# mLSTM attention and two dense layers on one core: how the first three tiles get their maxima, scores, states and weights

## The chip, the core and the metric

The kernel runs on one core of a Trainium2 chip (trn2). The metric is the device time of one execution in microseconds (us), of which three runs are shown. Below, PE is TensorE (PEld its weight loads), DVE is VectorE, ACT is ScalarE, POOL is GpSimd and SP is SyncE, which only issues transfers. "SPq" marks SP's queue.

## The reference

```python
B, H, S, D = 4, 8, 768, 40          # q, k, v, o_gate: (B, H, S, D); i_gate, f_gate: (B, H, S)
for t in range(S):
    m_new = np.maximum(f_gate[:, :, t] + m, i_gate[:, :, t])
    f_stab, i_stab = np.exp(f_gate[:, :, t] + m - m_new), np.exp(i_gate[:, :, t] - m_new)
    m = m_new
    C = f_stab * C + i_stab * (v_t outer k_t);   n = f_stab * n + i_stab * k_t
    y[:, :, t] = sigmoid(o_t) * (C @ q_t) / np.maximum(np.abs(n . q_t), 1.0)
x = y as (B*S, H*D) = (3072, 320)
x = np.maximum(x @ moe_w_in, 0.0) ** 2 @ moe_w_out            # w_in (320, 2048), w_out (2048, 320)
h = x @ moe2_w_in
out = np.where(h > 0.0, h, np.exp(np.minimum(h, 0.0)) - 1.0) @ moe2_w_out
```

All in float32.

## The kernel before

**Tiles.** The sequence is cut into 6 chunks of 128 steps; chunk c of batch b is tile g = 4c + b, 24 tiles of 128 tokens with 8 heads each. The recurrence is computed chunkwise. For each head there is a row m of running maxima (a scan over the gates on DVE). A tile needs its 8 rows of m on all 128 partitions, 1024 columns, in `wts[g % 3]`. ACT turns them into weights with one Exp of 128x128 for each head (`exponents`), POOL zeroes what lies above the diagonal (`mask`), PE forms the scores k·q (`scores`), DVE multiplies weights by scores (`weigh`), PE multiplies by v (`within`), DVE divides by the denominator and applies the output gate (`finish`), PE transposes the tile (`x1_transposed`), and ACT and DVE split it into a high and a low float32r part (`x_hi`, `x_lo`). The state at a chunk's end is the sum of k times `wv` (v weighted by the last column of the weights, `make_wv` on POOL, `state_added` on PE). Chunk 0 (tiles 0 to 3) has no state coming in; its sum is just copied (`first_state` on ACT). From tile 4 on there are also q and k splits and the state's share.

**Dense layers.** Three tiles (384 tokens) form a block, 8 blocks, two layers: 256 steps, t = 16·block + j, j a slice of 128 of the 2048 hidden columns. A step is `first_product(t)` (8 matmuls of 384 columns), the activation (ACT relu and square to `ghi`, POOL the full square `hact`, DVE the rest `glo`), and three steps later `second_product` (9 matmuls of 320 columns). PE's order is written out by hand, so is every other engine's; each engine runs its list in order and waits at semaphores.

**Prologue and block 0.** Tiles 0 to 2 must be done before step 0, since block 0 is made of them. The tiles of the next block are worked on between the steps of a block: tile g begins at step `start_of(g)` (tiles 3, 4, 5 and 6 at steps 0, 5, 10 and 15), with its matmuls at fixed offsets (scores at 0, state at 2, `within` at 3, transpose at 5).

**Weights.** Slice n of the first layer comes by SP as 128x704 words (352 KB) into a ring of four places. ACT makes the high part (`split_hi`, `split_out_hi`), DVE the low part of w_in (`split_lo`, two instructions) and POOL the low part of w_out (`split_out_lo`). Slices 0 to 3 are split in the prologue, slice t + 4 in step t. SP issues the load of slice n only when slice n - 4 is split, and that load stands in SP's list among the loads of q and k, v and the state, each with waits of its own.

**Maxima of the first tiles.** `spread_m` makes the rows of tiles 0 to 2 on PE: the maxima (32 rows) are multiplied with an identity column or with ones into PSUM, in the banks `acc` and `att`. Tiles from 3 on get them by a transfer: the maxima are written to DRAM (`m_rows`) and read back with the rows repeated on all partitions (`load_m`).

## Time and profile before

| | us |
|---|---|
| median of 3 runs | 877.79 (877.78 to 878.11) |
| the profiled execution | 878.74 |
| its span, first to last instruction | 877.0 |
| PE busy | 858.6 (98%) |
| DVE, ACT, POOL busy | 514.6, 436.7, 379.0 |

The span and the profiled time are 1.74 us apart. The stages are: the prologue up to step 0 at 50.73 us, block 0 up to 125.10 us, block 1 up to 183.37 us, and the other fourteen blocks. A row of the profile's views gives start and duration, engine, line of the kernel, operation, what it writes and reads, and at the end in brackets how long its engine had been idle and what released it.

### The profile page before, as it was taken

The page shows a single profiled execution, that of the slowest core. Times are in us where ns is not written, and L with a number is a line of the kernel's source. Part 1 is how long each engine was busy: PE and PEld are TensorE (multiplying, and loading weights), DVE is VectorE, ACT ScalarE, POOL GpSimd, SP SyncE. Part 2 cuts the span into 40 slices and gives each one's busy share as a digit, 9 for nine tenths or more (in the row PEclk, how much of TensorE's full clock was granted, in tenths as well). Part 3 has the DMA queues.
Part 4 walks back from the last instruction along what each step waited for, and adds up shares of the span by engine and source line. Part 5 has one row for each costly group of instructions (what it writes and reads, how often), then busy time and mean ns, then how long its engine had stood idle before and what let it go on. Part 6 is the DMA issues. An engine that isn't in the chain of part 4 may idle for free.

```text
span 877.0 us, 15290 instructions
## 1 busy us (share of the span) xinstructions
PE 858.6 (98%) x5633; PEld 838.5 (96%) x5633; DVE 514.6 (59%) x879; ACT 436.7 (50%) x955; POOL 379.0 (43%) x409
## 2 busy tenths in 40 slices
PE   9996899999999999999999999999999999999998
PEld 7876899999999999999999999999999999999998
DVE  4478888777678587775763764444444444444443
ACT  2274566465565565655734654434444443434343
POOL 2155564454444444543532754333334343433333
PEclk9997999999999999999999999999999999999999
DMA  6265443335354333453402410000000000000000
GB/s 166 82 213 178 133 104 100 99 104 135 90 162 108 101 99 100 108 135 102 130 4 96 117 50 1 16 10 13 11 2 23 1 23 1 24 1 23 1 24 24
DMA packets 21487, 63.86 MB, mean 73 GB/s; under 512 B 3012, under 2 KB 8996, under 8 KB 18852
## 3 DMA queue, kind: packets, MB, share of 16 engines
q1 hardware_dynamic: 21412, 62.88, 25.7%
q8 instruction: 45, 0.74, 0.4%
q14 instruction: 30, 0.25, 0.1%
HBM read 55.61 MB, written 4.03 MB: 68 GB/s over the span
## 4 chain that ended last, share of the span: by engine, by line
PE 91%; DVE 5%; DMA 1%; issue 1%; ACT 1%; POOL 1%; SPq 0%; DVEq 0%; ACTq 0%; POOLq 0%
PE hps L932 39%; PE acc L946 37%; PE att L849 4%; PE att L798 2%; PE att L841 2%; PE att L832 1%; PE att L854 1%; DMA x<-in_w_all 1%; PE acc L819 1%; DVE win L652 1%; PE hps L877 1%; PE att L855 1%; DVE win L651 1%; PE hps L798 0%; PE acc L807 0%
## 5 line engine op out<-in xcount | busy, mean ns | idle before, releaser
L932 PE MATMUL hps<-xth,win 128*128 128x384 f32 x1280 | 351.5, 340 | 2.2 <-DVE xtl L644 1.2
L946 PE MATMUL acc<-wout,ghi 128*128 128x320 f32 x1536 | 348.5, 313 | 0.0
L932 PE MATMUL hps<-xtl,win 128*128 128x384 f32 x768 | 260.2, 339 | 0.0
L946 PEld LDWEIGHTS acc<-wout,ghi 128*128 128x128 f32 x1536 | 259.0, 189 | 0.3 <-POOL glo L377 0.3
L946 PE MATMUL acc<-wout,glo 128*128 128x320 f32 x768 | 238.2, 310 | 0.0
L932 PEld LDWEIGHTS hps<-xth,win 128*128 128x128 f32 x1280 | 230.4, 189 | 3.0 <-DVE xtl L644 1.6
L377 POOL TENSOR_TENSOR glo<-hact,ghi 128x384 fp32r<-128x384 f32 x128 | 130.0, 1016 | 218.6 <-ACT ghi L544 218.6
L370 POOL TENSOR_TENSOR hact<-hact 128x384 f32<-128x384 f32 x128 | 109.5, 855 | 182.1 <-ACT hact L499 180.1
L748 DVE TENSOR_TENSOR glo<-hact,ghi 128x384 fp32r<-128x384 f32 x128 | 81.3, 635 | 116.1 <-POOL hact L370 115.8
L499 ACT ACTIVATE hact<-hps 128x384 f32<-128x384 f32 x128 | 62.7, 490 | 169.9 <-PE hps L932 169.9
L932 PEld LDWEIGHTS hps<-xtl,win 128*128 128x128 f32 x768 | 145.2, 189 | 0.0
L946 PEld LDWEIGHTS acc<-wout,glo 128*128 128x128 f32 x768 | 144.7, 188 | 0.0
L539 ACT ACTIVATE hact<-hact 128x384 f32<-128x384 f32 x128 | 67.3, 526 | 132.1 <-DVE hact L767 132.1
L767 DVE TENSOR_SCALAR hact<-hps 128x384 f32<-128x384 f32 x128 | 71.2, 556 | 104.0 <-PE hps L932 104.0
L770 DVE SCALAR_TENSOR_TENSOR hact<-hact,hps 128x384 f32<-128x384 f32 x128 | 70.9, 554 | 76.7 <-ACT hact L539 76.7
L544 ACT ACTIVATE ghi<-hact 128x384 fp32r<-128x384 f32 x128 | 67.2, 525 | 74.4 <-DVE hact L770 74.4
L502 ACT ACTIVATE ghi<-hact 128x384 fp32r<-128x384 f32 x128 | 67.1, 525 | 4.0
L301 POOL TENSOR_TENSOR q<-raw,q 40x512 fp32r<-40x512 f32 x40 | 57.4, 1453 | 11.2 <-ACT q L394 11.2
L418 ACT ACTIVATE wts<-wts,a_col 128x128 f32<-128x128 f32 x168 | 53.1, 388 | 0.0
L574 DVE RECIPROCAL gate<-gate 128x320 f32<-128x320 f32 x24 | 51.7, 2153 | 0.8
L849 PEld LDWEIGHTS att<-kvo,wts 128*128 128x128 f32 x352 | 43.9, 198 | 1.5 <-issue 1.5
L849 PE MATMUL att<-kvo,wts 128*128 128x41 f32 x352 | 43.0, 284 | 0.0
(151 smaller groups left out, 736.3 us busy)
## 6 DMA issues: line engine op xcount, KB each, us to landing
raw<-in_qk SPq DMA_DIRECT2D x20, 960.0 KB, 7.1
kvo<-in_kvo SPq DMA_DIRECT2D x23, 484.0 KB, 7.8
wts<-m_rows SPq DMA_DIRECT2D x21, 512.0 KB, 4.8
x<-in_w_all SPq DMA_DIRECT2D x16, 352.0 KB, 6.4
wts<-in_w_all SPq DMA_DIRECT2D x12, 352.0 KB, 3.0
out_x<-hsum SPq DMA_DIRECT2D x16, 160.0 KB, 1.9
state_rows<-state SPq DMA_DIRECT2D x40, 52.5 KB
kvo<-in_w_all SPq DMA_DIRECT2D x4, 352.0 KB, 4.4
```

Source lines behind the costliest of these rows:

```text
L370: nc.gpsimd.tensor_tensor(gfull[t % 2], relu[t % 2], relu[t % 2], ALU.mult).then_inc(s["g_ready"], 1)
L377: nc.gpsimd.tensor_tensor(glo[t % GR][:], gfull[t % 2], f32(ghi[t % GR][:]), ALU.subtract)\
L499: nc.scalar.activation(relu[t % 2], hps[t % 2][:, 0:NT], ACT.Relu).then_inc(s["relu_ready"], 1)
L502: nc.scalar.activation(ghi[t % GR][:], relu[t % 2], ACT.Square).then_inc(s["ghi_ready"], 1)
L539: nc.scalar.activation(relu[t % 2], relu[t % 2], ACT.Exp).then_inc(s["e_ready"], 1)
L544: nc.scalar.activation(ghi[t % GR][:], gfull[t % 2], ACT.Copy).then_inc(s["ghi_ready"], 1)
L748: nc.vector.tensor_tensor(glo[t % GR][:], gfull[t % 2], f32(ghi[t % GR][:]), ALU.subtract)\
L767: nc.vector.tensor_scalar(relu[t % 2], hps[t % 2][:, 0:NT], 0.0, None, ALU.min).then_inc(s["hneg_ready"], 1)
L770: nc.vector.scalar_tensor_tensor(out=gfull[t % 2], in0=relu[t % 2], scalar=-1.0, in1=hps[t % 2][:, 0:NT], op0=ALU.add, op1=ALU.max).then_i ...
L849: last = nc.tensor.matmul(bank[:, h * E:(h + 1) * E], wts[g % 3][:, h, :], v_of(g)[:, h, :], start=True, stop=True)
L932: last = nc.tensor.matmul(hps[t % 2][:, 0:NT], win[:, j, w, :], x[:, kk, :], start=(i == 0), stop=(i == len(parts) - 1))
L946: last = nc.tensor.matmul(acc[u][:, 0:DM], g[t % GR][:, cols], wout[:, j, w, :], start=(j == 0 and i == 0), stop=(j == NF - 1 and i == 2))
```

## The change

- Tiles 0 to 2 get their maxima by the transfer through DRAM too. `spread_m` and the `pick_m` of POOL are gone. ACT's `exponents` read them in place from `wts`.
- PE's prologue is in another order: the scores of tiles 0, 1 and 2 stand ahead of all `within`. Tile 2's scores go to `acc[0]`, `acc[1]`. The chunk-boundary maxima and the transposes of the inner part go to the free bank `acc[2]` instead of `hps[0]` and `att`. Of the 13 warming matmuls 8 are left, all at the start (before: 9, 1 and 3).
- `state_added(2)` moves from the prologue to step 1, `state_added(3)` to step 3; the last columns of the weights are kept by POOL (`keep_last`) and not by DVE, in one buffer for each tile.
- Tile 3 starts at step 1, tile 4 at 6, tile 5 at 11; tile 6 stays at 15.
- The ring has six places (`RING = 6`); slices 0 to 5 are split ahead of step 0 (`EARLY = 6`), their low part of w_in on POOL; in step t slice t + 6 is split. Slices 12 to 15 are loaded from ACT's queue in steps 2 to 5. SP issues slices 0 to 11 ahead of its step list. k, v and o of tiles 2 and 3 get buffers of their own.
- The output gate's 1 + e is made by ACT (Copy with bias) and not by DVE. `finish` stands one step earlier, behind `glo`.

```diff
-RING = 4
+RING = 6
+EARLY = 6
+POOL_LO = 6
+FROM_ACT = 12
+BEHIND = 2
+FIRST_STATES = {1: 2, 3: 3}
 def start_of(g):
-    return NF * (g // T - 1) + 5 * (g % T) - (g >= 2 * T)
+    if g < 2 * T:
+        return (1, 6, 11)[g - T]
+    return NF * (g // T - 1) + 5 * (g % T) - 1
...
+        def load_w(eng, n):
+            slot, loaded, _ = raw_w(n)
+            if n == RING - 3:
+                wait(eng, "s_ps", 4)
+            before = n - RING if n < NF else n - SPARE if n >= NF + SPARE else -1
+            if before >= 0:
+                win_lo_done(eng, before)
+                wait(eng, "wout_lo", before + 1)
+            eng.dma_start(slot, w_all[n // NF, n % NF]).then_inc(loaded, 16)
...
             for t in range((BLOCKS - 1) * NF):
-                if t + RING < NF:
-                    load_w(t + RING)
...
-            mask(0)
-            make_wv(0)
...
+            for g in range(T):
+                mask(g)
+                keep_last(g)
+                if g == 0:
+                    make_wv(0)
+            for n in range(EARLY):
+                if n == 4:
+                    make_wv(1)
+                    mask(T)
+                    keep_last(T)
+                if n < POOL_LO:
+                    split_lo(n)
+                split_out_lo(n)
             make_wv(2)
...
+            exponents(2, 1)
+            out_gate(1)
+            out_gate(2)
+            for n in range(2):
+                split_hi(n)
+                split_out_hi(n)
+            x_hi(0, 0, 0, A0)
+            for n in range(2, 4):
+                split_hi(n)
+                split_out_hi(n)
+            x_hi(1, 0, 1, A0)
+            first_state(0)
+            exponents(3, 0)
+            x_hi(2, 0, 2, A0)
+            exponents(3, 1)
+            first_state(1)
+            for n in range(4, EARLY):
+                split_hi(n)
+                split_out_hi(n)
+            out_gate(3)
...
-                        if t + RING < NF:
-                            split_hi(t + RING)
-                            split_out_hi(t + RING)
+                        if t + EARLY < NF:
+                            split_hi(t + EARLY)
+                            split_out_hi(t + EARLY)
+                        if FROM_ACT <= t + RING + EARLY - BEHIND < NF:
+                            load_w(act, t + RING + EARLY - BEHIND)
...
-                        g = tile_at(t, 4)
-                        if g is not None:
-                            finish(g)
...
+                        if t + EARLY < NF:
+                            split_lo(t + EARLY)
+                        g = tile_at(t, 3)
+                        if g is not None:
+                            finish(g)
```

PE's list from the first transpose to tile 2's scores (`ident` identity matrix, `raw` and one part of `x` hold q and k). Before:

```order
L883 MATMUL att<-ident,x 128x64
L877 MATMUL hps<-xth 128x384
L807 MATMUL acc<-x,ident 128x128 x8
L798 MATMUL att<-raw 128x128 x8
L819 MATMUL acc<-wts,hact 128x512
L819 MATMUL att<-wts,hact 128x512
L877 MATMUL hps<-xth 128x384 x3
L798 MATMUL hps<-x 128x128 x8
L819 MATMUL acc<-hact 128x512 x2
L849 MATMUL att<-kvo,wts 128x41 x8
```

and now:

```order
L895 MATMUL att<-ident,x 128x64
L829 MATMUL att<-raw 128x128 x8
L899 MATMUL att<-ident,x 128x128
L902 MATMUL acc<-ident,x 1x32
L903 MATMUL acc<-ident,x 1x128
L902 MATMUL acc<-ident,x 1x32
L903 MATMUL acc<-ident,x 1x128
L829 MATMUL hps<-x 128x128 x8
L908 MATMUL acc<-ident,hact 64x1
L909 MATMUL acc<-ident,hact 128x1
L829 MATMUL acc<-raw 128x128 x8
L861 MATMUL att<-kvo,wts 128x41 x8
```

Three groups that spread the maxima (L807 and L819 of before) and four warming matmuls are gone from between the scores; the boundary transposes moved up in their place.

SP's list from the load of slice 4 on, before (`in_w_all` is a weight slice, `in_qk` q and k of a tile, `state_rows` the state of one):

```order
L239 DMA x<-in_w_all 128x704
L208 DMA wts<-m_rows 128x1024
L239 DMA x<-in_w_all 128x704 x3
L218 DMA raw<-in_qk 120x2048
L239 DMA x<-in_w_all 128x704
L224 DMA kvo<-in_kvo 128x968
L232 DMA state_rows<-state 40x336
L232 DMA state_rows<-state 24x336
```

and now, from the load of slice 6 on:

```order
L236 DMA x<-in_w_all 128x704 x3
L246 DMA wts<-m_rows 128x1024
L236 DMA x<-in_w_all 128x704 x3
L257 DMA raw<-in_qk 120x2048
L265 DMA kvo<-in_kvo 128x968
L273 DMA state_rows<-state 40x336
L273 DMA state_rows<-state 24x336
```

Before, slice 9 stands behind the load of q and k of tile 5; now slices 0 to 11 all stand ahead of the first load of q and k with a state (tile 4), and none behind it.

POOL's list at the end of the prologue, from the weighted v of tile 1 on, before:

```order
L318 TENSOR_TENSOR wv<-kvo,last 128x328
L329 TENSOR_TENSOR wout<-x,wout 128x320
L318 TENSOR_TENSOR wv<-kvo,last 128x328
L329 TENSOR_TENSOR wout<-x,wout 128x320 x2
L306 AFFINE_SELECT wts<-wts 128x1024
L318 TENSOR_TENSOR wv<-kvo,wts 128x328
L370 TENSOR_TENSOR hact<-hact 128x384
```

and now:

```order
L351 TENSOR_TENSOR wv<-kvo,last 128x328
L339 AFFINE_SELECT wts<-wts 128x1024
L355 COPY last<-wts 128x8
L361 TENSOR_TENSOR win<-x,win 128x256
L363 TENSOR_TENSOR win<-x,win 64x128
L376 TENSOR_TENSOR wout<-x,wout 128x320
L361 TENSOR_TENSOR win<-x,win 128x256
L363 TENSOR_TENSOR win<-x,win 64x128
L376 TENSOR_TENSOR wout<-x,wout 128x320
L351 TENSOR_TENSOR wv<-x,last 128x328
L418 TENSOR_TENSOR hact<-hact 128x384
```

The mask of tile 3 now has two whole slices and tile 2's weighted v between itself and step 0's square.

## Rows read from the trace of the kernel before

**Rows 1.** Stages: length, busy PE, PEld, DVE, ACT, POOL, granted clock, DMA share, GB/s.
```profile
0.00:50.73 50.73, 47.15 (x202) 36.88 (x202) 25.76 (x66) 14.80 (x44) 11.09 (x22) 1.00 0.52 145
50.73:125.10 74.37, 63.45 (x416) 61.04 (x416) 62.46 (x96) 45.99 (x111) 45.10 (x43) 0.91 0.49 145
125.10:183.37 58.27, 58.27 (x428) 57.06 (x427) 42.45 (x67) 33.52 (x74) 27.34 (x28) 1.00 0.41 106
183.37:877.00 693.63, 689.72 (x4593) 683.57 (x4591) 383.96 (x652) 342.38 (x728) 295.47 (x316) 1.00 0.21 57
```

**Rows 2.** Waits of PE in block 0: total us, times, longest us.
```profile
PE att L854 <- DVE x L639: 10.9, 3, 6.7
```

**Rows 3.** Chain that ended last, prologue: start us, us, what.
```profile
5.61 3.71 PE acc L807 x16
9.32 3.71 PE att L798 x16
16.73 1.26 PE hps L877 x3
21.70 3.71 PE acc L819 x4
25.41 3.57 PE att L849 x16
29.23 1.25 PE att L832 x16
```

**Rows 4.** Timeline of PE around steps 0 to 6.
```profile
50.73 1.01 PE L932 MATMUL hps<-xth,win 128*128 128x384 f32 x2 [1.17 <-DVE xtl L644]
...
53.59 2.28 PE L798 MATMUL att<-x 40*128 40x128 f32 x16
...
64.16 0.51 PE L932 MATMUL hps<-xth,win 128*128 128x384 f32 x2
...
65.57 0.45 PE L946 MATMUL acc<-wout,ghi 128*128 128x320 f32 x2
...
66.89 0.51 PE L932 MATMUL hps<-xth,win 128*128 128x384 f32 x2
...
75.21 0.69 PE L854 MATMUL att<-ident,x 128*128 128x128 f32 x2 [6.74 <-DVE x L639]
```

**Rows 5.** Timeline of DVE, same stretch.
```profile
56.78 1.21 DVE L748 TENSOR_TENSOR glo<-hact,ghi 128x384 fp32r<-128x384 f32 x1 [4.06 <-POOL hact L370]
...
63.04 0.90 DVE L570 TENSOR_SCALAR gate<-gate 128x320 f32<-128x320 f32 x1
...
68.03 1.27 DVE L652 TENSOR_TENSOR win<-x,win 64x128 fp32r<-64x128 f32 x1
...
74.96 0.20 DVE L639 COPY x<-x 128x64 f32<-128x64 f32 x1
...
75.96 0.29 DVE L652 TENSOR_TENSOR win<-x,win 64x128 fp32r<-64x128 f32 x1
```

**Rows 6.** Timeline of ACT: eight exponents, and a wait for a slice.
```profile
51.44 2.44 ACT L418 ACTIVATE wts<-wts,a_col 128x128 f32<-128x128 f32 x8
...
79.27 0.52 ACT L442 ACTIVATE win<-x 128x384 fp32r<-128x384 f32 x1 [9.72 <-DMA x<-in_w_all]
```

**Rows 7.** Timeline of POOL.
```profile
51.26 0.87 POOL L329 TENSOR_TENSOR wout<-x,wout 128x320 fp32r<-128x320 f32 x1 [3.82 <-ACT wout L449]
53.95 1.09 POOL L306 TENSOR_SCALAR_AFFINE_SELECT wts<-wts 128x1024 f32<-128x1024 f32 x1 [1.83 <-ACT wts L418]
```

**Rows 8.** SP's queue, and its transfers of the maxima: us to landing.
```profile
4.52 0.33 SPq L249 DMA_DIRECT2D m_rows<-x  x1
...
DMA to landing us min/median/max: 8.1/8.1/8.1
...
71.14 0.35 SPq L218 DMA_DIRECT2D raw<-in_qk  x1
...
DMA to landing us min/median/max: 4.5/5.4/8.9
```

More of the change, by code:

```diff
@@ L89, in mlstm_two_dense_layers @@
         hsum = [sb(f"hsum_{i}", [P, H, E]) for i in range(2)]
-        gate = [sb(f"gate_{i}", [P, H, D]) for i in range(2)]
+        gate = [sb(f"gate_{i}", [P, H, D]) for i in range(3)]
         den = sb("den", [P, H])
@@ L132, in mlstm_two_dense_layers @@
             "x_whole x_ready rest_ready xt_ps xth_ready xt_ready h_ps relu_ready hneg_ready e_ready g_ready ghi_ready "
-            "glo_ready g_used acc_free win_hi win_lo wout_hi wout_lo out_done_0 out_done_1 out_done_2").split()
+            "glo_ready g_used acc_free win_hi win_lo win_lo_first wout_hi wout_lo out_done_0 out_done_1 out_done_2").split()
         s = {n: sem(n) for n in sem_names}
         m_in = [s[f"m_in_{i}"] for i in range(3)]
-        kvo_in = [s[f"kvo_in_{i}"] for i in range(2)]
-        w_in = [s[f"w_in_{i}"] for i in range(SPARE)]
+        kvo_in = [s[f"kvo_in_{i}"] for i in range(4)]
+        w_in = [s[f"w_in_{i}"] for i in range(RING)]
         out_done = [s[f"out_done_{i}"] for i in range(T)]
@@ L360, in _ @@
                             mask(g)
+                        if t == 2:
+                            make_wv(T)
                         g = tile_at(t, -2)
@@ L578, in weigh @@
                 dve.wait_ge(s["masked"], g + 1)
-                if g < T:
-                    wait(dve, "wv_ready", g)
-                    nc.vector.tensor_copy(last[:].unsqueeze(2), w[:, :, P - 1:P]).then_inc(s["last_ready"], 1)
+                if g < B:
                     dve.wait_ge(s["last_ready"], g + 1)
@@ L675, in _ @@
             summed(inner, every)
-            gate_plus(0)
-            gate_recip(0)
             highest(inner, every)
-            weigh(0)
-            gate_plus(1)
-            gate_recip(1)
-            weigh(1)
             dve.wait_ge(s["last_ps"], 1)
@@ L694, in _ @@
             nc.vector.tensor_copy(m0_line[:, 2:CH], m0_by_chunk[:, 1:CH - 1]).then_inc(s["m0_row_ready"], 1)
-            finish(0)
-            weigh(2)
+            gate_recip(0)
             dve.wait_ge(s["m0_ps"], 1)
-            nc.vector.tensor_copy(m0[0:2 * R, 0:1], hps[0][0:2 * R, 0:1])
-            step(nc.vector.tensor_copy(m0[:, 1:2], hps[0][:, 1:2]))
+            nc.vector.tensor_copy(m0[0:2 * R, 0:1], acc[2][0:2 * R, 0:1])
+            step(nc.vector.tensor_copy(m0[:, 1:2], acc[2][:, 1:2]))
             inner_m0, ends_m0 = m0[:, 1:2], m0[0:2 * R, 0:1]
@@ L896, in _ @@
-            state_added(0)
-            within(1)
-            pe.wait_ge(s["m_ready"], 2)
-            pe.wait_ge(s["p_ready"], 3)
-            for n in range(2):
-                nc.tensor.transpose(hps[0][0:1, n * R:(n + 1) * R], ends[0:R, 3 - n, P - 1:P], ident[0:R, 0:R])
-                done = nc.tensor.transpose(hps[0][0:1, 2 * R + n * P:2 * R + (n + 1) * P], inner[:, 3 - n, P - 1:P], ident[:])
-            done.then_inc(s["last_ps"], 1)
-            scores(2)
-            x1_transposed(0)
+            pe.wait_ge(s["a_ready"], 2)
@@ new lines, in _ @@
+            pe.wait_ge(s["a_col_ready"], 1)
+            nc.tensor.transpose(A2[:, 0:P], inner[:, 1, :], ident[:]).then_inc(s["a_ps"], 1)
+            pe.wait_ge(s["m_ready"], 2)
+            for n in range(2):
+                nc.tensor.transpose(acc[2][0:1, n * R:(n + 1) * R], ends[0:R, 3 - n, P - 1:P], ident[0:R, 0:R])
+                done = nc.tensor.transpose(acc[2][0:1, 2 * R + n * P:2 * R + (n + 1) * P], inner[:, 3 - n, P - 1:P], ident[:])
+            done.then_inc(s["last_ps"], 1)
+            scores(1)
@@ L911, in _ @@
+            scores(2)
+            within(0)
+            within(1)
+            x1_transposed(0)
             within(2)
             x1_transposed(1)
-            state_added(2)
+            state_added(0)
             pe.wait_ge(s["int_exp"], 1)
-            pe.wait_ge(s["den_ready"], 1)
-            nc.tensor.transpose(A1[:, 0:P], inner[:, 2, :], ident[:])
-            nc.tensor.transpose(A1[:, P:P + 2 * R], ends[:, 2, :], ident[0:2 * R, 0:2 * R])
-            nc.tensor.matmul(A1[0:D, 2 * P:3 * P], inner[:, 2, P - 1:P].broadcast_to([P, D]), ident[:], start=True, stop=True)\
+            nc.tensor.transpose(acc[2][:, 0:P], inner[:, 2, :], ident[:])
@@ L919, in _ @@
+            nc.tensor.transpose(acc[2][:, P:P + 2 * R], ends[:, 2, :], ident[0:2 * R, 0:2 * R])
+            nc.tensor.matmul(acc[2][0:D, 2 * P:3 * P], inner[:, 2, P - 1:P].broadcast_to([P, D]), ident[:], start=True, stop=True)\
                 .then_inc(s["int_ps"], 1)
             x1_transposed(2)
+            state_added(1)
             def first_product(t):
```

313 lines of the change are left out of this document (136 added, 177 removed).

## The prediction

> **What bounds the kernel now.** The windows of the stages come first [rows 1]. From 125 us on PE is busy in all of block 1 (58.27 of 58.27 us) and in 689.7 of the last 693.6 us at full granted clock, so no edit that only speeds another engine there can be seen. What is left is the front: 50.73 us until step 0, in which PE is busy too (47.15 us) but with work outside the dense layers, and block 0, which takes 74.37 us with PE busy for 63.45 and a mean granted clock of 0.91.
>
> The prologue next, in the chain that ended last [rows 3]: nearly all of it is PE. A group of 16 float32 instructions of 128 columns takes 3.71 us, the `within` groups 3.57 us, a state sum 1.25 us, and spreading the maxima costs 3.71 us for tile 0 and 3.71 us for tile 2. Tile 1's group lies between 13.03 and 16.73 us, also some 3.7 us: tile 0's scores end at 9.32 + 3.71 and the warming group begins at 16.73. These matmuls run at the lower clock: step 0's eight matmuls of 384 columns take from 50.73 to 53.59 us, and 1.41 us (64.16 to 65.57) once PE is at full speed [rows 4]. Columns by duration give the two levels, 1.2 and 2.4 GHz. The granted clock has no record before 54 us, so I go by those durations.
>
> Block 0 last. PE's waits there are three at the transposes of the tiles, 10.9 us in all, the longest 6.7 us [rows 2], up to 75.21 us [rows 4]. It waits for DVE's last instruction of `finish(3)`, which starts at 74.96 us. DVE had begun step 0 with `glo` at 56.78 us, released by POOL, and then worked without a pause: 18.4 us for what PE needs 11 to 12 us for [rows 5]. So DVE, started late and slow, bounds the first half of block 0. Beside it ACT waits 9.72 us for a weight slice until 79.27 us [rows 6]; that slice had stood in SP's queue behind the load of q and k issued at 71.14 us [rows 8], which itself waits for the splits. After each of the long waits PE runs at the lower clock for a time: the 0.91 of the stage is 0.09 × 74.37 = 6.7 us of full clock not given, of which PE had use for about 4.8 us (the rest fell into its wait).
>
> **Prologue, part by part.** Removed from PE's list: three spread groups, 3 × 3.71 = 11.1 us; the three warming matmuls 1.26 us [rows 3], the single one and one at the start by the same price 0.42 us each, 0.8 us; the state sum of tile 2, 1.25 us, moved to step 1. Together 14.4 us. Nothing is added to PE. As PE is busy in this stretch, what counts is whether the transfers are as fast as PE. Counted forwards: scores(0) needs q and k of tile 0, second in SP's list now instead of third, about 5.5 us (at most 7.3); then three score groups 11.1, three `within` 10.7, two state sums 2.5, and the small transposes, which I take unchanged, about 5: 5.5 + 29.3 = 34.8, and about 1 us for the last hand-over from PE to ACT to DVE before step 0 (now 1.17) [rows 4]. That gives 36, and backwards 50.73 - 14.4 = 36.3. I take step 0 at 36.0.
>
> What hides the transfers: the store of the maxima is issued at 4.5 us as before. Before it took 8.1 us to land [rows 8], with the loads of tiles 0 and 1 ahead of it in the queue; now 0.67 MB are ahead of it instead of 1.8 MB, and I take 2 to 3 us, with 8.1 as the upper end. The load of a tile's rows took 4.5, 5.4 and 8.9 us [rows 8]. Tile 0: 4.5 + 2.5 + 5.4 = 12.4 us; then eight exponents 2.44 [rows 6], mask 1.09 [rows 7], the last columns and the weighing about 1.6: 17.5 us. PE needs it for within(0) after three score groups and the transposes, at about 18. Tiles 1 and 2 follow at 512 KB plus 320 KB each; at the 145 GB/s of this stage [rows 1] that is up to 6 us each, 18.2 and 24 us for their landings, weighed by about 23.5 and 29; PE wants them at 22 and 27. A stage mean contains idle queues, so the true rate is above it; with a rate twice as high there are 2 to 3 us to spare. The cover is thin: each us that the first row comes later than 12.9 costs one. With the upper ends (4.5 + 8.1 + 8.9 = 21.5) step 0 is at 44.
>
> **Block 0, part by part.** Same PE work, plus the state sum of tile 2 at the upper clock, about 0.8 us with its issue. The wait that replaces the old one: POOL. Step 1 has `state_added(2)`, which needs `make_wv(2)`, and behind it on PE stand tile 3's scores and step 2. POOL masks tile 3 (1.09 us) when ACT has its second four exponents (about 36.7 us), keeps its columns (0.2), splits slices 4 and 5, each 0.87 us for w_out [rows 7] and by columns about 0.7 and 0.35 us for w_in, 1.9 us together, and then makes wv (0.75): 36.7 + 1.1 + 0.2 + 3.8 + 0.75 = 42.6 us. PE has done steps 0 and 1 at 36 + 2 × 2.6 = 41.2: a wait of 1.4 us. POOL's first square follows, and DVE's first `glo` starts at about 43.5 us, 7.5 us after step 0 instead of the 6.05 of before (56.78 - 50.73). From there DVE has the 18.4 us of before, less `gate_plus` 0.9 [rows 5], plus one step more of `glo` and a slice (tile 3 starts one step later), about 2.2: finish(3) is done at 63.2 us. PE gets to its transpose after seven first products (7 × 1.41 + 1.5 for the lower clock of the first = 11.4), three second ones (65.57 to 66.89 is 1.32 each, 4.0) [rows 4], the attention of tile 3 with scores 2.3 [rows 4] and 1.7 for within, two state sums 1.6, and the wait 1.4: 22.4 us, at 58.4. It waits 4.8 us instead of 6.7.
>
> After it, DVE needs about 20.7 us for the next five steps with tile 4, up to 83.9 us; PE has 5 × 2.73 + 4.7 = 18.4 us of work, 81.6: a wait of 2.3 us instead of about 3.5. The third wait (10.9 less 6.7 and 3.5, under 1 us) goes, since DVE catches up when no slices are left to split. ACT no longer waits for slices: 0 to 11 are issued by SP ahead of its steps, and the four loads on ACT's own list cost 0.35 us of issue each [rows 8] on an engine that is busy 46 of 74 us [rows 1]. That removal alone is worth little while DVE is the later one; its value is that PE isn't held twice. The lower clock after a wait of 4.8 us may come again; it delays PE by 2 to 3 us, and the second wait hides as much. From 83.9 us: 19.5 us to block 1's first product, 103.4. So block 0 takes 67.4 us, 7.0 less.
>
> Sum: 14.7 + 7.0 = 21.7 us. Blocks 1 to 15 unchanged. 878.74 - 21.7 = 857.0 for a profiled execution; the median of the runs lies 0.95 us under the profiled one, so **856.1, taken as 856.5**.
>
> **A rule against it.** POOL's new splits fall beside DVE's `finish` of tiles 0 to 2. On DVE the same 64x128 subtraction took 0.29 us alone (75.96) and 1.27 us beside POOL (68.03) [rows 5]. If each of the three multiplications of two SBUF operands in the prologue waits for one POOL instruction (0.87 us), that is 2.6 us on a chain with some 0.6 us to spare: step 0 at 38, and 858.5. The Trainium skill, SBUF — State Buffer, section Who interferes with whom, says that a VectorE instruction with two SBUF inputs and a GpSimd one that reads SBUF exclude each other for a whole instruction. These rows agree in direction. The range covers this case.
>
> **The rivals.** (a) As summed, one or two us either way: 0.50.
> (b) The front is shorter, but block 0 keeps its old length or gains only 2 us, since DVE begins 7.5 us behind and the waits grow instead of shrinking, with PE at the lower clock after them: 878.74 - 14.7 - 0 to 2, less 0.95: 861 to 863. For it: DVE's 62.46 busy us of 74.37 [rows 1] hardly change. 0.18.
> (c) Transfers late or DVE held: step 0 at 39 to 44, 859 to 865. 0.12.
> (d) DVE's slowness in block 0 was itself due to the bunching (1.27 against 0.29): with the slices of steps 0 to 3 already made and fewer waits, block 0 falls to 60 to 63 us of a PE sum of 57.5, 849 to 853. 0.15.
> (e) Slower. The maxima's transfers run one behind the other at their longest: 4.5 + 8.1 + 3 × 8.9 = 39.3 us for tile 2, then 6.5 us to weigh it, within, finish and transposes another 9: step 0 at 55, 4 us later than now, with no gain in block 0: 882. It decides from a landing of tile 2's rows at 35 us on. Against it: of the 8.9 most is time behind other loads. 0.02.
> (f) The change does nothing: PE's freed 14 us turn wholly into waits of the prologue, and block 0 stays: 877. It needs the first row at 27 us. 0.03.
>
> The range from 849.5 to 865 leaves out (e), (f) and some of the ends of (c) and (d). The likeliest case's own range is 853 to 859. The bound of a measurable difference is 0.2%, 1.8 us: faster 0.95, same 0.02, slower 0.03.
>
> **What the profile of the changed kernel would show.** PE's first product of step 0 at 36 us, with no wait over 1 us behind 12 us; the store of the maxima landed in under 3.5 us; ACT's first exponent at 12 to 13 us. PE waiting 1 to 2 us at step 1 for POOL's wv, 3 to 6 us at the first transpose, for DVE's `finish`, 1 to 3 at the second. No wait of ACT for a slice over 1 us. Block 1's first product at 103. Wrong if ACT waits for the maxima past 15 us, if the first transpose's wait is over 7 us, or if blocks 1 to 15 are not 751.9 us long again.

## The result, and the profile after

| | before | changed |
|---|---|---|
| median (4 runs each) | 877.95 us (877.78 to 878.78) | 867.25 us (867.17 to 868.81) |
| the profiled execution | 878.74 | 867.17 |
| its span | 877.0 | 865.4 |
| prologue, up to step 0 | 50.73 | 36.58 |
| block 0 | 74.37 | 76.91 |
| blocks 1 to 15 | 751.9 | 751.9 |

The ratio is 0.988, with a 95% interval of 0.9863 to 0.9898: 10.7 us faster, where 21.7 were forecast. The time lies outside the range given, above its upper end of 865. The prologue did what the prediction said, block 0 did not: it became 2.5 us longer, not 7.0 shorter.

The stages of the changed kernel, in the columns of [rows 1]:

```profile
0.00:36.58 36.58, 32.44 (x157) 28.53 (x157) 23.66 (x55) 18.60 (x53) 14.49 (x30) 1.00 0.82 269
36.58:113.49 76.91, 66.33 (x433) 63.89 (x432) 58.74 (x85) 46.33 (x109) 47.72 (x48) 0.91 0.49 134
113.49:171.79 58.30, 58.30 (x427) 57.09 (x426) 41.32 (x64) 34.92 (x77) 28.10 (x28) 1.00 0.36 98
171.79:865.40 693.61, 689.76 (x4593) 683.61 (x4591) 378.93 (x637) 348.81 (x742) 297.78 (x316) 1.00 0.20 57
```

Transfers in the prologue now run at 269 GB/s in the mean, where [rows 1] has 145; the prediction took 145 as a lower bound. In block 0 the mean granted clock is again 0.91, and PE is idle for 10.6 us where it was for 10.9.

The waits of PE from 30 to 130 us (total us, times, longest us), to be set beside [rows 2]:

```profile
PE att L866 <- DVE x L681: 8.6, 3, 5.7
PE att L844 <- POOL wv L351: 1.9, 1, 1.9
PE att L866 <- DVE xtl L686: 1.3, 2, 1.0
```

There are still three waits at the transposes, and the one for POOL's weighted v at step 1 has joined them (the last row, for the low part of a finished tile, belongs to the end of the prologue). In order of time, from PE's timeline (start us, us, then what; in brackets the idle time before it and what ended it):

```profile
36.58 1.01 PE L935 MATMUL hps<-xth,win 128*128 128x384 f32 x2
...
43.61 0.81 PE L844 MATMUL att<-wv,x 128*40 128x41 f32 x16 [1.94 <-POOL wv L351]
44.35 3.70 PE L829 MATMUL att<-raw 40*128 40x128 f32 x16
47.98 1.01 PE L935 MATMUL hps<-xth,win 128*128 128x384 f32 x2
...
69.07 0.69 PE L866 MATMUL att<-ident,x 128*128 128x128 f32 x2 [5.65 <-DVE x L681]
...
92.05 0.44 PE L866 MATMUL att<-ident,x 128*128 128x128 f32 x2 [1.45 <-DVE x L681]
...
109.58 0.44 PE L866 MATMUL att<-ident,x 128*128 128x128 f32 x2 [1.53 <-DVE x L681]
```

Tile 3's scores took 3.70 us here and 2.28 in [rows 4]. The windows of these stretches (columns as in [rows 1]) show why:

```profile
44.50:51.20 6.70, 6.70 (x26) 6.48 (x27) 5.77 (x8) 0.77 (x3) 3.50 (x4) 0.50 0.43 113
51.30:68.30 17.00, 12.12 (x90) 11.50 (x89) 15.63 (x15) 12.85 (x30) 14.57 (x14) 1.00 0.84 239
68.40:75.10 6.70, 6.03 (x24) 6.03 (x25) 5.03 (x12) 1.65 (x5) 0.00 (x0) 0.50 0.56 180
```

The granted clock is 0.50, the level of 1.2 GHz, from 44.5 us on, 0.9 us behind the end of the wait of 1.94 us, and again from 68.4 us on, when most of the wait of 5.65 us has passed.

And DVE, which PE waits for at 69.07 us. Its timeline from the first `glo` (L780) to the last instruction of `finish(3)` (L681); L693 and L695 are the low part of a slice, L629 the weighing, L614 the low part of k:

```profile
44.38 1.20 DVE L780 TENSOR_TENSOR glo<-hact,ghi 128x384 fp32r<-128x384 f32 x1 [7.37 <-POOL hact L418]
...
52.38 0.56 DVE L780 TENSOR_TENSOR glo<-hact,ghi 128x384 fp32r<-128x384 f32 x1 [1.99 <-POOL hact L418]
...
58.79 1.91 DVE L614 TENSOR_TENSOR k<-raw,k 40x1024 fp32r<-40x1024 f32 x1
60.73 3.59 DVE L780 TENSOR_TENSOR glo<-hact,ghi 128x384 fp32r<-128x384 f32 x1
64.24 2.68 DVE L693 TENSOR_TENSOR win<-x,win 128x256 fp32r<-128x256 f32 x1
66.95 0.29 DVE L695 TENSOR_TENSOR win<-x,win 64x128 fp32r<-64x128 f32 x1
67.27 0.17 DVE L668 TENSOR_SCALAR den<-att 128x8 f32<-128x8 f32 x1
...
68.83 0.20 DVE L681 COPY x<-x 128x64 f32<-128x64 f32 x1
```

From 44.38 to 68.83 us are 24.5 us; the prediction had 19.7. Three things in these rows more than fill the difference of 4.8 us: 1.99 us in which DVE had nothing to do, since step 2 came late on a slow PE; `glo` of 3.59 us, which takes 0.56 at 52.38 us; and a slice's low part of 2.68, which takes 0.42 where it is shortest here. Together they are 7.3 us over the short values; the 18.4 us of before, from which the 19.7 came, had some stretched instructions in them too, such as the 1.27 us of [rows 5]. Last, POOL at that moment (L334 splits q, L418 is the square):

```profile
59.65 3.46 POOL L334 TENSOR_TENSOR q<-raw,q 40x512 fp32r<-40x512 f32 x2
63.08 0.82 POOL L418 TENSOR_TENSOR hact<-hact 128x384 f32<-128x384 f32 x1
63.86 1.17 POOL L376 TENSOR_TENSOR wout<-x,wout 128x320 fp32r<-128x320 f32 x1
65.00 0.82 POOL L418 TENSOR_TENSOR hact<-hact 128x384 f32<-128x384 f32 x1
65.78 0.85 POOL L376 TENSOR_TENSOR wout<-x,wout 128x320 fp32r<-128x320 f32 x1
```

The slow `glo` ends 1.2 us behind POOL's two subtractions, and the slow L693 (64.24 to 66.92 us) lies beside the instructions that follow them. All of `finish(3)` stands behind them in DVE's list, although what it needs, the sums of `within(3)`, PE had ended by 57.9 us.

### The profile page after: what moved, and what is told of

It reads as the page before. It is cut to its first block, busy times and chain, and to the rows that moved or that the text cites. A ratio compares the mean times of both kernels' runs of the same rounds, so it can differ in the third digit from the quotient of the medians.

```text
span 865.4 us, 15226 instructions
## 1 busy us (share of the span) xinstructions
PE 846.8 (98%) x5604; PEld 833.1 (96%) x5604; DVE 502.6 (58%) x839; ACT 448.7 (52%) x980; POOL 388.1 (45%) x422
## 4 chain that ended last, share of the span: by engine, by line
PE 89%; DVE 5%; issue 2%; DMA 2%; POOL 1%; ACT 1%; SPq 0%; DVEq 0%; POOLq 0%
PE hps L935 40%; PE acc L949 38%; PE att L861 4%; PE att L829 2%; PE att L853 2%; PE att L866 1%; PE att L844 1%; DMA wts<-m_rows 1%; DVE glo L780 1%; DVE gate L618 1%; DVE win L693 1%; PE att L867 1%; DVE win L695 1%; POOL hact L418 0%; ACT wts L463 0%
## 5 line engine op out<-in xcount | busy, mean ns | idle before, releaser
L418 POOL TENSOR_TENSOR hact<-hact 128x384 f32<-128x384 f32 x128 | 112.7, 881 | 196.2 <-ACT hact L546 194.6
L780 DVE TENSOR_TENSOR glo<-hact,ghi 128x384 fp32r<-128x384 f32 x128 | 87.8, 686 | 134.8 <-POOL hact L418 134.0
L334 POOL TENSOR_TENSOR q<-raw,q 40x512 fp32r<-40x512 f32 x40 | 58.6, 1484 | 8.7 <-ACT q L442 8.4
L463 ACT ACTIVATE wts<-wts,a_col 128x128 f32<-128x128 f32 x192 | 60.5, 388 | 3.3 <-DMA wts<-m_rows 3.3
L339 POOL TENSOR_SCALAR_AFFINE_SELECT wts<-wts 128x1024 f32<-128x1024 f32 x24 | 26.2, 1094 | 37.0 <-ACT wts L463 37.0
L861 PEld LDWEIGHTS att<-kvo,wts 128*128 128x128 f32 x336 | 42.0, 198 | 0.4 <-issue 0.4
```

Of the source, the lines that this page charges most:

```text
L418: nc.gpsimd.tensor_tensor(gfull[t % 2], relu[t % 2], relu[t % 2], ALU.mult).then_inc(s["g_ready"], 1)
L780: nc.vector.tensor_tensor(glo[t % GR][:], gfull[t % 2], f32(ghi[t % GR][:]), ALU.subtract)\
L861: last = nc.tensor.matmul(bank[:, h * E:(h + 1) * E], wts[g % 3][:, h, :], v_of(g)[:, h, :], start=True, stop=True)
```

## The experiments

A stretched instruction below is one that takes longer than the same instruction does at other places of the same kernel. The theories, by what they say (the expectations give them letters, and those of the last four kernels give the letters anew): **the order**, that DVE's list holds `finish(3)` back behind `glo` and slices; **the clock**, that the wait for POOL at step 1 puts PE at 1.2 GHz and so makes DVE's input late; **the neighbour**, that POOL's subtractions stretch DVE's instructions. The expectations have one more for the fall of the clock, S: not the wait but tile 3's scores behind it bring it down. The sums by stage, all from the profiled executions; "DVE's chain" is the time from the start of the first `glo` to that of the last instruction of `finish(3)`:

| kernel | ratio, 95% interval | step 0 at | block 0 | DVE's chain |
|---|---|---|---|---|
| changed, once more | 0.9852 (0.9817, 0.9886) | 37.0 | 76.7 | 24.2 |
| finish first | 0.9787 (0.9754, 0.982) | 37.0 | 69.1 | 15.4 |
| wv(2) early | 0.9818 (0.979, 0.9846) | 36.3 | 74.2 | 20.6 |
| low parts 4, 5 on DVE | 0.9814 (0.9799, 0.9829) | 36.6 | 72.7 | 21.4 |
| q's low part on DVE | 0.9819 (0.9783, 0.9855) | 37.1 | 77.6 | 21.0 |
| warming at step 1 | 0.9835 (0.9801, 0.9869) | 35.4 | 73.4 | 21.5 |
| four slices early | 0.9871 (0.9855, 0.9888) | 38.0 | 78.4 | 24.7 |
| tiles a step earlier | 0.9827 (0.9785, 0.9868) | 35.7 | 73.4 | 18.2 |
| slices from the step list | 0.9995 (0.9976, 1.0014) | 37.0 | 89.3 | 31.7 |
| three-part | 0.9746 (0.9731, 0.976) | 37.6 | 66.5 | 19.1 |
| three-part, once more | 0.9743 (0.972, 0.9766) | 37.4 | 67.1 | 15.3 |
| three-part and q on DVE | 0.9769 (0.9748, 0.9789) | 36.9 | 69.7 | 16.6 |

The changed kernel's first ratio is 0.988, its second 0.9852. The experiments ran in three groups, and the kernel before, measured with each, did not take the same time in all: 880.2 us beside finish first, wv(2) early, q's low part and warming; 879.04 beside the changed kernel once more, low parts 4 and 5, four slices early and three-part; 878.85 beside the other four. So between groups the ratios are compared and not the times. Against the two ratios of the changed kernel, finish first gains 0.65 to 0.93% (5.7 to 8.2 us); wv(2) early, low parts 4 and 5 and q's low part each gain 0.33 to 0.66% (2.9 to 5.8 us), and warming 0.17 to 0.45% (1.5 to 4.0 us). The intervals of these last four overlap with the changed kernel's second one, that of finish first overlaps with it in its uppermost part.

**The changed kernel once more**, unedited, as the base of comparison.

> The changed kernel itself, unedited, as the measure for the runs beside it on this chip, since the kernel before ran at 880.2 us on the chip of the first four experiments instead of 877.95. All theories: ratio to the kernel before 0.986 to 0.990, with the wait at step 1 and the lower clock behind it in the profile.

866.22 us, but four runs from 861.42 to 868.78; the ratio of 0.9852 is just under the 0.986 to 0.990 expected. In its profile DVE's chain is 24.2 us long like the first time, though `glo` at the place of the first time's 3.59 us took 1.22 us. DVE was idle three times (2.58, 0.85 and 1.43 us), and PE had the lower clock for a longer stretch:

```profile
44.10:54.20 10.10, 10.10 (x48) 9.58 (x48) 6.68 (x10) 3.37 (x10) 5.50 (x7) 0.50 0.52 127
```

The stretched instruction is there too, only it is the next one of DVE's list, again beside POOL's two subtractions for q:

```profile
63.46 2.75 DVE L693 TENSOR_TENSOR win<-x,win 128x256 fp32r<-128x256 f32 x1
63.08 2.84 POOL L334 TENSOR_TENSOR q<-raw,q 40x512 fp32r<-40x512 f32 x2
```

So which instruction is stretched changes from run to run, and how much of the chain is stretching and how much idle time; the length of the chain hardly did between these two. As four runs of one kernel lie up to 7.4 us apart, a single profile can't price an edit of 1 to 3 us.

**Finish first.**

```diff
                             update_state(g)
                             add_inter(g)
+                            finish(g)
...
-                        g = tile_at(t, 3)
-                        if g is not None:
-                            finish(g)
```

Both pieces stand in DVE's step list: `finish(g)` moves ahead of this step's `glo`, nothing else changes.

> Against the changed kernel (span 865.4 us, step 0 at 36.58, block 1 at 113.49). DVE's finish of a tile is put ahead of glo and the slice of the same step. Theory L (DVE's list and its length set the end of finish(3)): finish(3) no longer waits for glo(4) 3.59 us and the slice's 2.68 and 0.29 us, so x_ready comes about 6 us earlier, at 62.5, PE's 5.7 us wait at the first transpose goes and with it the lower clock after it: block 1 5 to 9 us earlier, 857 to 861 us of time. Theory C (it is the clock lost at step 1 that counts): the wait only moves to glo(3) or glo(4) needed by a second product, gain under 2 us.

861.74 us (859.09 to 863.12). DVE's timeline at the place of before:

```profile
57.16 1.22 DVE L614 TENSOR_TENSOR k<-raw,k 40x1024 fp32r<-40x1024 f32 x1
58.42 0.17 DVE L668 TENSOR_SCALAR den<-att 128x8 f32<-128x8 f32 x1
...
60.17 0.75 DVE L681 COPY x<-x 128x64 f32<-128x64 f32 x1
60.84 0.55 DVE L781 TENSOR_TENSOR glo<-hact,ghi 128x384 fp32r<-128x384 f32 x1
61.31 1.51 DVE L693 TENSOR_TENSOR win<-x,win 128x256 fp32r<-128x256 f32 x1
```

and PE's waits up to 130 us:

```profile
PE att L842 <- POOL wv L351: 3.0, 1, 3.0
PE att L864 <- DVE xtl L686: 1.3, 2, 1.0
PE att L864 <- DVE x L681: 1.2, 2, 0.7
PE att L842 <- DVE xtl L686: 1.0, 1, 1.0
```

The wait at the first transpose is gone, and with it 7.6 to 7.8 us of block 0, although the wait for POOL was longer here (3.0 us) and PE ran 6.6 us at 0.50 behind it. The profiled execution is the fastest of the four, 2.6 us under their median; by the ratios the gain is 5.7 to 8.2 us, still the largest of any single edit. So the order is the largest part of the loss, and the early dip of the clock alone doesn't hold block 0 up. The edit does one thing more: DVE's `finish(3)` is over at 60.92 us, just when POOL's subtractions for q begin (60.83 us), so the instructions that they stretch now stand behind it. What the order is worth has the neighbour's share in it.

**The weighted v of tile 2 early.** POOL's `make_wv(2)` moves from behind slices 4 and 5 to ahead of them.

```diff
                     keep_last(T)
+                    make_wv(2)
...
-            make_wv(2)
```

> POOL makes tile 2's weighted v ahead of slices 4 and 5. Both theories: PE's 1.9 us wait at step 1 goes. Theory C (that wait drops the clock from 44.5 to 51.3 us): no lower clock after step 1, scores of tile 3 in 1.9 instead of 3.7 us, step 2 at 43.5 to 45 instead of 47.98, DVE's 2.0 us wait at 52.4 gone, time 3 to 5 us less. Theory S (it is the float32 scores, with few columns for their time, that let the clock fall): the lower clock comes anyway and the gain is 1 to 2 us. Theory L: whatever comes earlier on PE is lost again at the first transpose, under 1.5 us in all.

864.16 us (863.79 to 864.42). The wait at step 1 is gone, and so is the fall of the clock behind it; PE's wait at the first transpose is larger than in the changed kernel, and the clock falls in it:

```profile
39.10:62.90 23.80, 18.34 (x140) 16.96 (x138) 18.56 (x19) 17.59 (x42) 20.44 (x24) 1.00 0.61 182
63.00:73.10 10.10, 7.69 (x30) 7.69 (x31) 6.63 (x17) 2.85 (x9) 1.83 (x2) 0.50 0.81 215
...
PE att L866 <- DVE x L681: 9.4, 3, 6.5
```

The clock theory is right on the cause of the early dip (no wait, no dip); S is refuted, for tile 3's scores take 2.05 us here and the clock stays up behind them. DVE's chain is 3.6 us shorter than in the repetition, although a slice's low part in it took 3.54 us beside POOL's subtractions. But PE arrives earlier too and gives 0.9 us of it back in the wait. Block 0 gains 2.5 to 2.8 us, the whole 3.0 to 5.4 us by the ratios.

**The low parts of slices 4 and 5 on DVE** (`POOL_LO = 4` in place of 6), which brings POOL's weighted v forward as well and gives DVE four instructions more.

> The low w_in parts of slices 4 and 5 are made by DVE, which is idle from 37 to 44 us, and not by POOL; four POOL instructions of 0.73 and 0.46 us go, about 2.5 us, ahead of tile 2's weighted v. Theory C: the wait at step 1 goes and with it the lower clock after it, as with POOL's reordering, and in addition POOL's first square comes 2.5 us earlier and so does DVE's glo: first glo at 42 instead of 44.4. Gain 3 to 5 us against the changed kernel. Theory L alone (DVE's chain from its first glo on sets the first transpose): gain 2 to 2.5 us, just the earlier start.

862.41 us (861.55 to 863.04). The first `glo` starts at 42.09 us and not at 44.38; PE waits 1.1 us at step 1, and the clock doesn't fall behind it; the wait at the first transpose is 6.3 us, and block 0 gains 4.2 us. This one act of the change, two slices' low parts put on POOL, cost more than it brought: DVE was idle for 7.37 us ahead of the first `glo` in the changed kernel.

**Warming products in the wait.** Eight products of zeros at step 1, ahead of the state sum, so that PE is idle for less of the wait.

```diff
+                    if t == 1:
+                        pe.wait_ge(s["decay_ready"], 1)
+                        keep_warm(8)
                     if t in FIRST_STATES:
                         state_added(FIRST_STATES[t])
```

> Eight matmuls of 384 columns on zeros, into a bank not in use, fill PE's 1.9 us wait at step 1; nothing else is moved. Theory C: the clock stays up, scores of tile 3 take 1.9 us, step 2 starts at 46 instead of 47.98 and finish(3) about 2 us earlier, time 2 to 4 us less. Theory S: the clock falls in the scores all the same, time within 1 us of the changed kernel or up to 1 us longer.

865.38 us (862.55 to 866.16). The granted clock is 1.00 from 39.3 to 63.0 us here too: of the wait at step 1 the eight products leave 0.90 us, and the clock doesn't fall. Block 0 takes 73.4 us, with a wait of 5.8 us at the first transpose. It agrees with wv(2) early by another way: what the early dip costs block 0 is some 3 us in the profiles. But the profiled execution is the fastest of its four, 2.8 us under their median, and by the ratios the gain is 1.5 to 4.0 us, which the spread of the changed kernel's runs hardly lets one tell from nothing.

**q's low part on DVE**, as one instruction of 40x1024 in place of POOL's two of 40x512, for tiles from 4 on.

> The low part of q of every tile from 4 on is made by DVE in one instruction of 40x1024 instead of POOL in two of 40x512. Theory P (DVE's instructions are held by POOL's long q split: glo(4) took 3.59 us and the w_in subtraction 2.68 us beside it, against 0.55 and 0.42 us alone): both return to under 1.3 us, finish(3) ends 3 to 4 us earlier although DVE has 1.2 us more work, time 2 to 5 us less. Theory L0 (those two durations are no lock but waiting for something of their own): no gain, or 1 us more from DVE's added work.

863.16 us (863.06 to 867.58). DVE's timeline:

```profile
58.32 1.22 DVE L610 TENSOR_TENSOR k<-raw,k 40x1024 fp32r<-40x1024 f32 x1 [0.98 <-ACT k L433]
60.97 1.22 DVE L783 TENSOR_TENSOR glo<-hact,ghi 128x384 fp32r<-128x384 f32 x1 [1.43 <-POOL hact L414]
62.11 1.04 DVE L693 TENSOR_TENSOR win<-x,win 128x256 fp32r<-128x256 f32 x1
```

Without POOL's subtractions for q, no subtraction in the chain takes over 1.3 us, and PE waits 2.28 us at the first transpose where it waited 5.65 (its longest wait is now the one for POOL at step 1, 3.0 us). Wherever one of these kernels has POOL split q inside DVE's chain, one subtraction beside it takes 2.3 us or more: 3.59 and 2.75 in the changed kernel, 3.54 with wv(2) early, 2.71 with low parts 4 and 5, 4.35 with warming, 2.71 with four slices, 2.31 a step earlier, 3.32 with SP's list, 2.29 in the first three-part profile. That supports the neighbour theory. In the kernel before, though, the longest beside POOL's split of q is 1.51 us. The block's 77.6 us in the table come from the profiled execution, which is the slowest of the four (the other three are at 863.1). It has a third stretch at the lower clock, from 107.3 to 114.2 us; that the others lacked it is likely from their times but not shown, as they have no trace. By the ratios the neighbour costs about as much as the early dip.

**Only four slices ahead of step 0** (`EARLY = 4`, `POOL_LO = 4`), as before the change.

> Only slices 0 to 3 are split ahead of step 0, slice t + 4 in step t (its w_in low part on DVE) as in the kernel before; the ring keeps six places. POOL has two slices less ahead of the first square (4.3 us), DVE 1.5 us more in steps 0 to 11 each later slice at its place. If the two early slices paid: 1 to 3 us slower than the changed kernel. If what POOL does between the mask of tile 3 and step 0's square costs more (theory C and late start of DVE): 2 to 4 us faster, first glo at 40 to 41 us and no wait at step 1.

867.82 us (866.52 to 870.03). No gain: `x1_transposed(3)` waits 7.6 us, the others 3.8 us together, and ACT is late once (1.2 us). The first `glo` came at 42.26 us, yet DVE's chain took 24.7 us. It holds as many slices as in the changed kernel; DVE was idle in it for 5.6 us, 3.48 of them for ACT's high part of k, and one slice's low part took 2.71 us. Splitting six slices early is neither the loss nor much of a gain.

**Tiles 3 to 5 one step earlier** (steps 0, 5, 10 in place of 1, 6, 11).

> Tiles 3, 4 and 5 start at steps 0, 5 and 10 in place of 1, 6 and 11; all else as in the changed kernel. Theory C (block 0 has its waits where other engines' work is not there yet, and TensorE has only a step or two of other work to lay over them): GpSimd's make_wv(2) ends at 43.5 us and TensorE would want it from about 37.6 us on, so the wait for it grows from 1.9 us to 5 to 6 us; the wait at the first transposition falls from 5.7 us to 1 to 3 us, since VectorE's chain has the same start (the first glo) and TensorE comes to it later; sum of the waits unchanged, 865 to 869 us. Rival (theory L, the length of block 0 is a sum of lateness at the first transposition alone): starting a step earlier takes 4 us or more off, 863 us or less.

863.94 us (860.48 to 868.94). My forecast of the waits was wrong on one side: PE waits 0.31 us for tile 2's `wv` and 1.73 for tile 3's, and not 5 to 6, because tile 3's scores now lie between step 0 and step 1 and cover the first. The wait at the first transpose is 2.28 us, within the 1 to 3 expected, and that at the second 3.01 us. The time lies between the two theories' figures, and the spread of 8.5 us over four runs decides nothing.

**The slices from SP's step list**, one a step, as before the change; no loads from ACT's queue.

```diff
-FROM_ACT = 12
+FROM_ACT = 99
...
-            for n in range(RING, RING + 3):
-                load_w(sp, n)
             load_m(4)
-            for n in range(RING + 3, FROM_ACT):
-                load_w(sp, n)
             load_qk(4)
 
             for t in range((BLOCKS - 1) * NF):
+                if t + RING < NF:
+                    load_w(sp, t + RING)
```

> The changed kernel with the first block's weight slices 6 and on issued one a step from SyncE's list, as in the other blocks, and none from ScalarE's queue. In the profile of the changed kernel no engine waits for a weight slice in block 0. If the place from which the slices are issued decides nothing, the time is that of the changed kernel, a ratio of 0.983 to 0.988, with no wait for win or wout over 1 us. Rival (transfers issued a step ahead of use come too late behind the queries, keys and gates of the queue, the price of the change's early issues): waits for win of 1 us or more for several steps in block 0, and 870 us or more.

879.27 us (875.44 to 881.47): the whole gain is gone, as the rival had it. ACT's timeline of the waits for slices, and SP's queue (start us, us, what it issued):

```profile
54.81 0.52 ACT L485 ACTIVATE win<-x 128x384 fp32r<-128x384 f32 x1 [13.64 <-DMA x<-in_w_all]
81.45 0.52 ACT L485 ACTIVATE win<-x 128x384 fp32r<-128x384 f32 x1 [9.47 <-DMA x<-in_w_all]
```

```profile
47.02 0.35 SPq L257 DMA_DIRECT2D raw<-in_qk  x1
47.48 0.81 SPq L236 DMA_DIRECT2D x<-in_w_all  x2
...
73.19 0.35 SPq L257 DMA_DIRECT2D raw<-in_qk  x1
73.63 0.35 SPq L236 DMA_DIRECT2D x<-in_w_all  x1
```

Slices 6 and 7 leave at 47.48 us, as soon as the load of q and k ahead of them in the queue may go. This is the wait of [rows 6] and [rows 8] again, and larger. With step 0 14 us earlier than in the kernel before, it reaches PE: 6.4 us of waiting for ACT's `hact`, since ACT's list is stopped at the slice. So the new place of the weights' loads is worth 12.4 us of block 0 (89.33 less 76.91), once the prologue is short, and 10.1 to 12.6 us by the ratios. How this divides between SP's early issues and ACT's queue is open, since the edit takes both back. The profile of the changed kernel can't show that, because the wait is not there.

**Three parts together:** finish first, `make_wv(2)` early, and slices 4 and 5's low parts on DVE.

> Three edits together: finish ahead of glo, tile 2's weighted v ahead of slices 4 and 5, and those slices' w_in low parts on DVE. Theory L and C both: no wait at step 1, full clock from 39 us on, first glo 1.6 us earlier, finish(3) at 58 to 60 us against a PE arriving at 57.5 to 58.5: first wait under 2 us, no lower clock in block 0, block 1 at 101 to 104 us instead of 113.5, time 854 to 858 us by this chip's measure (ratio to the kernel before 0.971 to 0.976). If the waits only move on to tiles 4 and 5: 859 to 862.

856.8 us (854.7 to 857.06), the fastest of all and 1.1% under the changed kernel beside it. PE has no wait at step 1, and the first transpose waits 4.1 us. The time is as expected; the wait (under 2 us) and the clock (no fall in block 0) are not:

```profile
37.58:104.09 66.51, 61.61 (x433) 59.34 (x432) 60.68 (x89) 46.23 (x109) 45.52 (x44) 0.95 0.56 155
...
60.60:67.20 6.60, 4.77 (x20) 4.77 (x21) 6.34 (x15) 2.60 (x8) 2.95 (x4) 0.50 0.86 196
...
PE att L864 <- DVE x L681: 4.8, 2, 4.1
PE att L864 <- DVE xtl L686: 1.3, 2, 1.0
```

> The three-part kernel once more, as the base for the kernel with q's low part moved, and for how far one kernel's times lie apart between chips or batches: 856.8 us and a ratio of 0.9746 before. If the gain is the order of the work and not a lucky clock, the ratio is within 0.973 to 0.977 and the lower clock stands in one stretch of 6 to 8 us of block 0; if it was luck of the clock, it rises to 0.980 or more with two such stretches.

857.39 us (856.15 to 857.49), a ratio of 0.9743 against 0.9746: it is the order and no luck of the clock. Its profile had other waits (none at the first transpose, 2.3 us for q's split behind it, 0.45 and 0.72 us at the other two transposes), one stretch at the lower clock (61.9 to 68.9 us) and the same length of block 0 within 0.6 us, so 66 to 67 us is what this order gives whichever engine is a little late.

**Three parts, and q's low part on DVE.**

> The three-part kernel (finish(g) ahead of glo, make_wv(2) ahead of slices 4 and 5, their low parts on DVE) with q's low part moved from GpSimd to VectorE as well, one 40 x 1024 operation a tile in place of two of 40 x 512. In the changed kernel glo(4) took 3.59 us and the product next to it 2.68 us while GpSimd's subtraction for q took 3.46 us; with q on VectorE alone the changed kernel went to a ratio of 0.9819. Theory C (what is left of the first wait is VectorE's backlog between the first glo and finish(3)): finish(3) now stands ahead of glo, so the 1.2 to 2.3 us of q's subtraction lie ahead of it or behind it with little gain, the wait of 4.1 us at the first transposition stays at 3 to 5 us, and the time is within 2 us of the three-part kernel in this batch. Rival (theory P, GpSimd holds VectorE up throughout): the wait falls under 2.5 us and the time falls by 3 us or more against the three-part kernel.

859.49 us (857.98 to 859.92), 2.1 us slower than the three-part kernel beside it. The wait at the first transpose is 1.55 us. That decides nothing, since the three-part kernel had 4.1 us there in one profile and none in the other. But PE now waits for DVE's q:

```profile
PE att L830 <- DVE q L614: 3.8, 2, 2.9
PE att L867 <- DVE x L681: 3.6, 2, 2.1
```

The wait is what the rival expected (under 2.5 us), but the time did not fall; it lies at the edge of what the first theory expected (within 2 us). Once `finish` stands first, taking work from POOL to the engine that is late buys nothing.

## Why the prediction was wrong, point by point

**The prologue, right in its length.** Step 0 at 36.58 us, forecast 36.0. The store of the maxima landed 2.0 us after its issue (forecast under 3.5), and ACT had its first maxima at 13.46 us (forecast 12 to 13). PE's longest wait there for a transfer is 1.2 us, for q and k. The path is less right. The prediction reads nearly all of the old prologue's chain as PE's; the whole chain up to step 0 has 34.4 us of PE and 13.4 us of DVE, most of it at the end (the `finish` of tiles 0 to 2). In the changed kernel that chain has 4.5 us of PE, 12.1 of DVE and 13.1 of transfers, 8.83 us of these for tile 1's maxima, landed at 16.2 us and not at 18. So step 0 at 36.6 agrees with a sum of PE's work of 36.3 us, but the last to be ready were the maxima and then DVE: the cover that the prediction calls thin was just enough. The lower clock of the prologue, which the prediction takes from durations, is on record in other profiles: with wv(2) early the granted clock is 0.50 from 10.0 to 39.1 us.

**The rule against it, at the other place.** The 2.6 us that DVE might have lost to POOL in the prologue did not come: step 0 is not at 38. In block 0 they did: `glo` of 3.59 us beside POOL's 3.46 us, and no subtraction over 1.3 us in that chain when this work was not on POOL. The Trainium skill, SBUF — State Buffer, section Who interferes with whom, says that a VectorE operation with two SBUF inputs contends with a GpSimd one that reads SBUF; the rows agree, and `glo` was stretched over more than one of POOL's instructions (two in 3.46 us).

**The wait for POOL at step 1, right:** 1.94 us against 1.4, and the first `glo` at 44.4 against 43.5 us. What I did not carry on is what this wait does to the clock. The sum up to the first transpose has the lower clock only as 1.5 us for step 0's product, and nothing for it behind the wait. There it stood for 6.7 us in which PE was busy, 3.4 us lost, with scores(3) at 3.70 us and step 2 not ended before 52.4. The 1.5 us are too little as well: with them steps 0 and 1 are 2 × 1.41 + 1.5 = 4.3 us, while the same prediction had counted 2 × 2.6 us for them a few lines before, and they took 5.1. PE so came to the first transpose 26.8 us after step 0, forecast 22.4.

**The step that failed: DVE's 19.7 us from the first `glo` to `finish(3)`,** which were 24.5 (release at 69.07 against 63.2 us; 32.5 us after step 0 and not 27.2). Of the 9.5 us by which block 0 came out longer than the 67.4 forecast, 5.3 lie here and 4.2 behind the first transpose. I took the 18.4 us of before as a fixed amount of work. It is a list with `finish(3)` behind whatever `glo`, slice and split are late, and the experiments show its length between 15.3 and 31.7 us. The order alone changes it from 24 to 15 us: one `glo` and one slice (4.9 us in the repetition, 2.75 of them one stretched instruction) now stand behind `finish(3)`, and the idle time in the chain falls from 4.9 to 0.9 us. I named `finish` standing behind `glo` in the change, and put no price on it.

**The second step that failed: "the second wait hides as much".** From the first transpose to block 1 I had 40.2 us; they were 44.4. The lower clock from 68.4 to 75.1 us was not hidden: with PE busy for 6.03 us at half speed it is 3.0 us lost, and behind it the second and third waits came nevertheless (1.45 and 1.53 us, forecast 2.3 and none).

**"That removal alone is worth little", wrong in what it says of the weights.** Put back under the new prologue, the old place of the loads costs 12.4 us. The sum was not hurt by this, since I had ACT's wait gone.

**Rival (b) was the case that came,** and worse than I had it: block 0 even grew by 2.5 us, so 867 and not 861 to 863. Its reasoning (DVE begins late, waits grow, the clock falls behind them) is what the rows show. Against its condition I held that DVE's backlog would shrink by the slices already made; that is true for the work (58.74 us busy instead of 62.46) and wrong for the place of `finish` in it. The forecast's 67.4 us of block 0 is what the three-part kernel gives (66.5 and 67.1), some 10 us less than the changed kernel's, from edits that I had not seen as needed; that the two figures agree is luck. The chances had a slip as well: (e) at 0.02 and (f) at 0.03 don't fit slower 0.03 and same 0.02.

**What stays open:** how the loss divides between the clock and the neighbour. Each alone brings some 3 us by the ratios or the profiles, the two overlap in the same stretch, the order has part of the neighbour in it, and the changed kernel's own runs spread over 7.4 us. That the spread itself is the clock's doing fits the two profiles but wasn't tried.

## What to carry to other kernels

When a wait moves or a start comes earlier, a late engine's time up to the released instruction is not a constant: write out its list, find what stands ahead of the instruction that the bounding engine waits for, and ask whether it must; putting it first was worth more here than any other single edit tried. Price a new wait of the bounding engine at the wait plus the stretch at the lower clock behind it, unless rows show that stretch idle anyway. And a cure for a stall that costs nothing now may be what carries the next gain: test it under the new timing, not under the old.

## What the runs showed of the hardware

- Where PE was idle for 1.9 to 3.0 us at step 1 (changed kernel, its repetition, finish first, q's low part on DVE, SP's list), the granted clock went to 0.50 for 3.5 to 10.3 us, from the wait's end to 2.4 us behind it. Where it was idle there for 1.1 us (low parts 4 and 5), 0.90 us (warming) or not at all (wv(2) early, four slices, three-part), the clock stayed at 1.00 until the wait at the transpose of tile 3 or, in the three-part repetition, the wait for q of 2.3 us behind it, some 20 us later; a wait of 1.47 us at step 3 with wv(2) early did not bring it down. With tile 3 a step earlier it fell behind a wait of 1.73 us.
- The same kernel's runs differ more than expected when such waits are near: 861.4 to 868.8 us for the changed one, 854.7 to 857.5 over eight runs of the three-part one.
- One DVE subtraction of 128x384 took 0.49 us at best (low parts 4 and 5 on DVE) and 3.59 us beside POOL (changed kernel), and the one of 40x1024 for k took 1.22 us and, in the kernel with warming, 4.35. Beside POOL's two subtractions for q (2.6 to 3.5 us together) one DVE subtraction took 2.3 to 4.35 us in ten profiles, and no more than 1.51 us in two (the kernel before and finish first); the `glo` of 3.59 us ended 1.2 us behind the second of them.
